# Turning 18 token tiles through DRAM and VectorE's 32 by 32 transpose instead of TensorE, in a kernel of pooled attention and a channel mix

## The reference, cut to what matters

```python
def _attn_ref(q, k, v):                       # q, k, v: 4 x 8 x 1152 x 64
    q_pool = q.reshape(B, H, S // 2, 2, D).mean(axis=3)
    scores = scale * np.matmul(q_pool, k.transpose(0, 1, 3, 2))
    attn = np.exp(scores - np.max(scores, axis=-1, keepdims=True))
    attn = attn / (np.sum(attn, axis=-1, keepdims=True) + 1e-09)
    return np.matmul(attn, v)

def _moe_ref(x, g_ln, w_ch1, w_ch2):          # x: 4 x 576 x 512, w_ch1: 512 x 2048
    mu = np.mean(x, axis=-1, keepdims=True)
    var = np.mean((x - mu) ** 2, axis=-1, keepdims=True)
    xn = (x - mu) / np.sqrt(var + 1e-06) * g_ln
    return x + np.maximum(xn @ w_ch1, 0.0) @ w_ch2
```

## Time and profile before

| what | us |
|---|---|
| median of 3 runs | 806.26 (805.49 to 806.8) |
| the profiled execution: device time | 805.31 |
| the profiled execution: span of the core | 803.5 |
| TensorE busy in the span | 792.1 (99%) |
| VectorE busy | 640.5 (80%) |
| ScalarE busy | 417.4 (52%) |
| POOL busy | 446.0 (56%) |
| DMA traffic | 75.36 MB, mean 94 GB/s |

### The profile page before, as it was taken

The page is one execution under the profiler, slowest core; times in us unless marked ns, Lnnn a source line. Parts: engine busy times, 40 slices in busy tenths (PEclk is TensorE's granted clock), DMA queues, the critical chain, the costliest instruction groups (busy, mean ns, idle before and its releaser), DMA issues. The chain is left out here.

```text
span 803.5 us, 17054 instructions
## 1 busy us (share of the span) xinstructions
PE 792.1 (99%) x6472; PEld 662.9 (83%) x6472; DVE 640.5 (80%) x991; ACT 417.4 (52%) x941; POOL 446.0 (56%) x341
## 2 busy tenths in 40 slices
PE   8999999999999999999999999999999999999998
PEld 6778777787778777788879999989899989999897
DVE  6987889888889989888597767898867888766654
ACT  4677556576556675667723354543244444333431
POOL 3899989888888888787795221331411342131100
PEclk9999999999999999999999999999999999999999
DMA  8566634466534565311112211214212122422112
GB/s 193 130 146 147 143 97 97 105 148 147 119 89 103 131 148 141 69 67 44 32 53 66 93 53 53 66 53 138 85 66 69 58 72 66 154 70 64 55 40 79
DMA packets 39681, 75.36 MB, mean 94 GB/s; under 512 B 8880, under 2 KB 23472, under 8 KB 36016
## 3 DMA queue, kind: packets, MB, share of 16 engines
q1 hardware_dynamic: 38128, 73.88, 35.0%
q10 hardware_dynamic: 1472, 0.39, 0.3%
HBM read 69.54 MB, written 4.72 MB: 92 GB/s over the span
## 5 line engine op out<-in xcount | busy, mean ns | idle before, releaser
L588 POOL TENSOR_TENSOR acc<-acc,pT 128x576 f32<-128x576 f32 x160 | 240.7, 1505 | 23.2 <-ACT pT L932 0.4
L1299 PE MATMUL banks<-w2f,hT 128*128 128x512 f32 x864 | 214.3, 393 | 0.0
L932 ACT ACTIVATE pT<-banks 128x576 f32<-128x576 f32 x288 | 171.8, 658 | 37.0 <-PE banks L726 31.4
L1299 PEld LDWEIGHTS banks<-w2f,hT 128*128 128x128 f32 x864 | 160.3, 188 | 28.8 <-issue 0.2
L1043 DVE TENSOR_REDUCE pm<-banks 128x2 f32<-128x1024 f32 x128 | 153.4, 1222 | 37.5 <-PE banks L672 36.0
L728 PE MATMUL banks<-qT,kT 64*128 64x288 f32 x1728 | 162.0, 298 | 2.4 <-DVE pm L1043 1.8
L728 PEld LDWEIGHTS banks<-qT,kT 64*128 64x128 f32 x1728 | 133.9, 184 | 17.2 <-DVE pm L1043 7.3
L739 PE MATMUL banks<-pT,vn 128*64 128x288 f32 x1152 | 146.1, 408 | 0.0
L1377 ACT ACTIVATE hT<-mid 128x384 fp32r<-128x384 f32 x88 | 46.4, 527 | 182.0 <-DVE mid L1444 181.0
L398 POOL TENSOR_TENSOR w_sums<-w_stage 128x256 f32<-128x256 f32 x22 | 17.7, 806 | 210.9 <-DMA w_stage<-in_moe_w_ch_dram 210.9
L1444 DVE TENSOR_TENSOR mid<-banks,mid 128x384 f32<-128x384 f32 x154 | 85.5, 555 | 59.2 <-PE banks L1288 55.9
(11 more groups left out here) (122 smaller groups left out, 960.9 us busy)
## 6 DMA issues: line engine op xcount, KB each, us to landing
q_in_rows<-in_q_dram SPq DMA_DIRECT2D x56, 284.0 KB, 6.6
k_in_rows<-in_k_dram SPq DMA_DIRECT2D x56, 284.0 KB, 5.1
w_stage<-in_moe_w_ch_dram SPq DMA_DIRECT2D x24, 512.0 KB, 3.8
w_stage<-in_moe_w_ch_dram SPq DMA_DIRECT2D x48, 256.0 KB, 2.7
vn<-in_v_dram SPq DMA_DIRECT2D x16, 576.0 KB, 4.7
out_dram<-x SPq DMA_DIRECT2D x16, 256.0 KB, 3.1
q_in_rows<-in_q_dram SPq DMA_DIRECT2D x4, 256.0 KB, 3.0
k_in_rows<-in_k_dram SPq DMA_DIRECT2D x2, 288.0 KB, 4.0
```

Source lines behind the costliest of these rows:

```text
L588: nc.gpsimd.tensor_tensor(total, pT[:, h % 2, 0] if kt == 1 else total, pT[:, h % 2, kt], ALU.add).then_inc(chained, 1)
L932: nc.scalar.activation(pT[:, h % 2, kt], pair_banks("S", n)[:, :, 0:HW], ACT.Exp, scale=SCALE).then_inc(exp_done, 1)
L1299: last = nc.tensor.matmul(banks[:, k % 2 * (CT // 2) + kk], hT[:, k, a, tokens], w2f[:, (2 * u + k // 2) % 4, b], start=p == 0 and k < 2 a ...
```

## The change

1. TensorE's transpositions of tokens are gone, in attention and in the mix, with the waits around bank 7.
2. In their place, for each tile: SP sends the normalised tile to a DRAM tensor `tokens` (`send_tokens`, 128 rows of 2 KB); when it has landed, SP fetches it with four DMAs of 64 KB (`fetch_blocks`), each to 32 partitions, in pieces of 32 float32 numbers (128 bytes), so that the 32 by 32 blocks stand in transposed places; when these have landed, VectorE turns each block in itself with one STREAM_TRANSPOSE of 128 x 512 (`turn_tokens`), into `xg_a` or `xg_b`. ScalarE multiplies there in place by g (`scale_tokens`). The blocks use the memory of `token_sums`, in three sets.
3. The order of normalising, of the statistics (now two tiles at a time in the units 2 to 4 for the third part, its moments at the end of unit 9), of the power on POOL (one unit earlier) and of the work of the last two pairs of attention on VectorE and ScalarE moves accordingly. The high parts of the forms B12 and B22 of the first part go from VectorE to ScalarE.
4. At the start: 8 of the 28 idle transpositions go, one group of maxima goes ahead of the keys of the second pair, and the second piece of the first keys is loaded by SP behind the first instead of by ScalarE's queue.

```diff
-                  "S@6 M@4 S@0 O@6 E@3 L@0 T@4 PV@2 T@0 KQ@4 KA@6 SH@3 Z@1 PV@0")
+                  "S@6 M@4 S@0 O@6 E@3 L@0 PV@2 KQ@4 KA@6 SH@3 Z@1 PV@0")
-    FIRST_STEPS = "KQ@2 W@7 W@7 KA@0 W@7 M@4 M@6 M@4 W@2 M@6 W@2 M@4 KA@0 M@6 M@2 KQ@4 L@6 W@1 W@1 SF@0"
+    FIRST_STEPS = "KQ@2 W@7 KA@0 M@4 M@6 M@4 W@2 M@6 W@2 M@4 M@6 KA@0 M@2 KQ@4 L@6 W@1 W@1 SF@0"
...
-        def turn_tokens(n, kk, bank):
-            nc.tensor.wait_ge(xn_ready, CT * n + kk + 1)
-            for c in range(DC):
-                last = nc.tensor.transpose(bank[:, c * 128:(c + 1) * 128],
-                                           xn[:, kk % 2, c * 128:(c + 1) * 128], ident[:])
-            last.then_inc(xn_turned, 1)
+        def blocks(t):
+            at = t % BLOCK_SETS * DM
+            return token_sums[:].rearrange("p s c w -> p (s c w)")[:, at:at + DM]
+
+        def send_tokens(sp, n, kk):
+            t = CT * n + kk
+            sp.wait_ge(xn_ready, t + 1)
+            sp.dma_start(tokens[t], xn[:, kk % 2]).then_inc(xn_sent[t % 2], 16)
+
+        def fetch_blocks(sp, n, kk):
+            t = CT * n + kk
+            sp.wait_ge(xn_sent[t % 2], 16 * (t // 2 + 1))
+            wait(sp, tokens_turned, t - BLOCK_SETS + 1)
...
+            for r in range(128 // BLOCK):
+                sp.dma_start(blocks(t)[r * BLOCK:(r + 1) * BLOCK].rearrange("j (c a i) -> j c a i", c=DC, i=BLOCK),
+                             tokens_v[t, r]).then_inc(blocks_in[t % BLOCK_SETS], 16)
+
+        def turn_tokens(n, kk):
+            t = CT * n + kk
+            nc.vector.wait_ge(blocks_in[t % BLOCK_SETS], 64 * (t // BLOCK_SETS + 1))
...
+            nc.vector.transpose(half[:, :, at].rearrange("p c (a j) -> p c a j", j=BLOCK),
+                                blocks(t).rearrange("p (c a i) -> p c a i", c=DC, i=BLOCK)).then_inc(tokens_turned, 1)
...
             first_keys(sp, 0, k_first)
+            first_keys(sp, 1, k_in)
...
-            first_keys(act, 1, k_in)
...
             for u in range(UNITS):
+                n, p = u // FP + 1, u % FP
+                if n < PARTS:
+                    if p == 2:
+                        send_tokens(sp, n, 0)
+                        send_tokens(sp, n, 1)
+                        fetch_blocks(sp, n, 0)
+                        fetch_blocks(sp, n, 1)
+                    elif p in (3, 4):
+                        fetch_blocks(sp, n, 2 * p - 4)
+                        send_tokens(sp, n, 2 * p - 3)
+                        fetch_blocks(sp, n, 2 * p - 3)
                 if u + 2 < UNITS:
                     load_first_weights(sp, u + 2)
...
                 if p == 1 and n > 1:
+                    moments_of(n)
+                    variance_eps(n)
+                if p in (2, 3, 4):
+                    turn_tokens(n, 2 * p - 4)
+                if p in (2, 3):
+                    normalize(n, 2 * p - 2)
+                if 2 <= p < 5 and n + 1 < PARTS:
                     dve.wait_ge(x_written, PAIRS)
-                    for kk in range(4):
-                        statistics(n, kk)
...
-                if p == 2 and n > 1:
-                    statistics(n, 4)
-                    statistics(n, 5)
-                    moments_of(n)
-                    variance_eps(n)
-                if p in (4, 5):
-                    normalize(n, 2 * p - 5)
+                if p == 2:
+                    normalize(n, 0)
+                    normalize(n, 1)
+                if p in (3, 4, 5):
+                    turn_tokens(n, 2 * p - 5)
+                if p in (3, 4):
+                    normalize(n, 2 * p - 3)
```

135 lines of the change are left out of this document (74 added, 61 removed).

## The result

The changed kernel takes 797.38 us, the median of 4 runs (796.51, 797.13, 797.62, 800.43), against 806.0 for the kernel before, the median of its 4 runs. The ratio is 0.9896, 95% interval 0.9881 to 0.9911: 1.0% faster. The forecast was 796.0, its range 794.4 to 799.2. The profiled execution took 796.51 us with a span of 794.8 (before 805.31 and 803.5), so it gained 8.8 us where the sum had 10.3.

What follows compares the result with a forecast made beforehand. TensorE's instruction stream was taken as the bound; gains of 5.3 + 3.8 + 0.8 + 0.4 = 10.3 us, added work hidden, bring 805.3 to 795.0 profiled, 796.0 in the median; 8-in-10 range 794.4 to 799.2.

Steps and rivals of the forecast that it cites:

- forecast case: Whole kernel: the summed gains arrive and the added work stays hidden; 794.5 to 797 us, chance 0.66.
- first rival: Units 2 to 5 and 10: VectorE becomes the bound, costing 3.0 us, so 799.0 us; chance 0.18.
- Transpositions in the mix: Mix: removing 12 tile transpositions at 0.44 us each from TensorE's path gains 5.3 us.
- the statistics: Unit 10: moving the third part's statistics to units with room removes the excess over 15.65 us, gaining 0.8 us.
- Transpositions in attention: Attention: three pairs that turn two tiles each lose 1.27 us at their ends, gaining 3.8 us.
- The start: Program start: four fewer idle transpositions let the first keys be turned sooner, and every later step follows; 0.4 us gained.
- SP's queue: Unit 2: unit 4's first weights, behind sends and fetches, land by 460.8 us plus queueing; 2.3 us to spare, cost nothing.
- Attention keeps its time: Attention's last pairs: late fetches delay maxima twice by 1.3 us, or ScalarE's casts hold the end; 798.6 us, chance 0.06.
- VectorE at nothing: VectorE: 18 added transpositions, 0.65 us each by length, fit its idle time; units 3 and 4 reach 13.5 and 14.9 us busy.
- The way through DRAM: Mix: a tile's send and fetches take 7.3 to 9.5 us, hidden with 0.5 us to spare at the slow end.
- Room on the DMA engines: DMA engines: a tile's 2048 pieces at 22.7 ns take at most 2.9 us, so there is room enough.
- third rival: SP's queue, units 2 to 4 and 10 to 12: small pieces clog the DMA engines, up to 819 us; chance 0.06.

Runs made afterwards that it cites:

- Putting the price back: Changed kernel with four idle TensorE transpositions at each of the 12 places of the mix where a tile was turned before; 806.29 us.
- six-fetch run: Changed kernel with six small fetches instead of four for each of the mix's 12 tiles, VectorE waiting for them too; 807.62 us.
- two kernels with the old list: Changed kernel with the earlier first steps, 797.17 us; the same with last values loaded sooner and one GpSimd add fewer in attention's last half, 797.26 us.
- run with the 2.6 us wait: Changed kernel with the keys of the second pair turned ahead of the sixth group of maxima again; 800.56 us.

## Why the prediction was right, and where it was off

The mechanism of the main sum is shown: what left TensorE's stream left the time. The measured median, 797.38, lies just above the band of the forecast case (794.5 to 797) and in that of the first rival (797 to 799.5), but not by that rival's mechanism: the 1.5 us between sum and profile are the start and the last pair. Of the signs of being right, the units 3 to 5 and 10 to 13 (15.6 to 15.7 us), the ends of the pairs 12 and 13 (10.8 us) and TensorE's waits (8.3 us in total) came as stated.

*Transpositions in the mix, 5.3, and the statistics, 0.8:* right; 6.21 us measured for 6.1. Putting the price back gave 6.4 for the 5.3 (1.0 of it unexplained), and the statistics alone gave their 0.8 in the kernel before.

*Transpositions in attention, 3.8:* right; 3.77. No run put these back; the stretch of the pairs 11 to 14 alone shows it. Comparing the ends of two pairs, instead of counting 2 x 0.44, was what made it so.

*The start, 0.4 gained:* wrong, 0.37 lost in the profiled execution, 0.1 to 0.5 over all profiles at full clock. The step that failed is "Every later step of the start waits for this one". The first maximum did come 0.38 us sooner. But the keys of the second pair already bound the start of the kernel before: they were turned at 13.89, 0.13 us behind their landing. In the change their load is issued 0.23 us sooner, but lands only 0.10 sooner. And the change puts a group of maxima ahead of them, which the prediction gave no price at all; they are turned at 14.47. With the order put back they are turned 0.13 us behind their landing again, never before 13.98, and the first scores follow 5.8 us behind that. That they land 0.1 to 0.3 us later in those runs than at 13.76 isn't explained. A stretch with two inputs gains only what both gain.

*The last pair, costed at nothing:* 0.76 lost. What failed is an omission: SP's queue was followed past the weights of the mix, and not past `load_values(PAIRS - 1)`, which went from 0.44 us behind the end of pair 14 to 8.13 behind it. By itself that made TensorE wait 0.9 us. Taking it away didn't bring the time back, since the turns and the waits for blocks also delay VectorE's low parts and, beside these, GpSimd's sum (26.9 for 26.4). Of the rival "Attention keeps its time" this is what came: nothing in pairs 12 to 14, 0.8 us at the end, and in the changed kernel not by ScalarE's casts.

*VectorE at nothing:* right. 0.70 us a turn, and 8.4 us more of them cost 0.45. Its busy time was counted 1.2 us too high in each unit (12.27 for 13.5 in unit 3, 13.66 for 14.9 in unit 4). The second part of the first rival, that GpSimd's adds stretch two-operand work of VectorE, occurs (4.15 us for two low parts that take 0.95 each elsewhere), and the kernel before had it in the mix too: in unit 4 a `hidden_lo` took 1.09 us and a low part of a weight 0.97 beside GpSimd's sums. With the change's order no `hidden_lo` of that unit takes more than 0.60 us and no low part of a sum more than 0.43, which is most of the 1.2 us. That was luck: the prediction did not see it.

*The way through DRAM:* right for the mix. A send and a fetch land after 2.6 us each (3 to 5 was the sign for the small pieces), and VectorE never waits for blocks there. In the last pair, which the prediction did not follow, it waits 3.0 and 1.9 us for them.

*Room on the DMA engines:* right, with the bound on the high side. In the stretch from 448.2 to 454.5 us, nearly all of it two tiles' fetches (packets, MB, share of 16 engines),

```profile
q1 hardware_dynamic: 3713, 0.57, 50.9%
```

are 0.509 x 6.3 x 16 / 3713 = 13.8 ns a packet, where 22.7 was the bound: 1.8 us of the 16 engines for a tile and not 2.9. (This takes in 59 packets of 2048 bytes; by themselves the packets of 128 bytes average 12.9 ns over the whole run.) The Trainium skill's 512 bytes ("DMA: Bandwidth & Descriptors", Specifications) doesn't decide here: pieces of 128 bytes are indeed slow for their size, 128 bytes in 13.8 ns being 9.3 GB/s for an engine where the 2048-byte packets of this stretch take 86.5 ns, or 23.7 GB/s, but a tile is 2048 of them and no more. A read-modify-write no row here shows.

*SP's queue:* right, and closely. The first weights were to land at 460.8 in the time of the kernel before, with 2.3 us to spare. They landed at 458.34; this place stands 2.6 us earlier now (454.73 for 457.30), so 460.9 by the old time. The six-fetch run puts the room at 2.1. The third rival's sign, ScalarE's casts waiting for their weights in the units 3 and 11, did come (2.9 us in each), and cost nothing: as a sign it was too sharp, since ScalarE has that time to spare. The six-fetch run also shows how near that rival was: 1.3 us more of SP a tile turned a gain of 8.8 us into a loss of 1.8 (one execution, with one stretch at the lower clock in it).

## What to carry to other kernels

When a step is taken off the engine that bounds the kernel, its price can be read from two equal stretches with and without it, and in a steady loop it comes back whole. Where the program changes phase, several inputs arrive just in time, so a sooner one gains nothing until the others are followed too: go through every queue that the new instructions join, list what stands behind them, and find for each step the input that lands last. Many small DMAs may cost the issuing queue more than the DMA engines; the thing to compare is the seconds of issue, here 0.65 us for 64 KB, with the slack of the load behind them.

## What the runs showed of the hardware

*The clock at the start.* The changed kernel ran once with the first scores at 20.08 us and once at 21.94, with the same instructions. In the second run, by stretches (PEclk is the column ahead of the DMA share):

```profile
9.00:12.00 3.00, 2.04 (x12) 1.02 (x12) 2.62 (x3) 2.39 (x7) 0.92 (x1) 1.00 0.80 204
12.00:16.00 4.00, 4.00 (x16) 2.51 (x15) 3.86 (x4) 0.00 (x0) 4.00 (x3) 0.52 0.93 211
16.00:19.00 3.00, 3.00 (x19) 2.55 (x17) 1.65 (x2) 1.93 (x2) 0.57 (x1) 0.51 0.96 197
```

TensorE had idled 0.9 us for VectorE's maxima in the first of these, then the clock fell to the 1.2 GHz level at 12.14 us and rose at 18.97. The run with idle transpositions in the mix shows the same at 11.73 to 18.56. Both have the shortened list of first steps; so do other profiles at full clock, with the same idle 0.9 us, so that idle time alone doesn't decide it. Whether the removed idle transpositions make this likelier is open: eight runs of the two kernels with the old list (796.2 to 798.2) and eight of the changed kernel (796.3 to 800.4) are too few.

*Short waits can cost more than themselves.* TensorE's waits for the last values of 0.9, 1.7, 1.8 and 2.15 us were followed by no lower clock. The waits of 2.6 us there and of 2.4 us in the mix were each followed by 3.4 us at the 1.2 GHz level. The changed kernel's run of 800.43 us has no profile; its mean granted clock, 0.998, is that of the run with the 2.6 us wait (800.56 us), so it may be the same case, which is not shown.

*GpSimd and VectorE slow each other.* One GpSimd add of 128x576 takes 1.4 us, and a low part of VectorE's with two SBUF operands 0.95. Side by side either gets longer: at 390.45 us, after, an add took 2.29 us while the low part beside it kept its 0.94, and from 407.78 on two low parts took 2.05 and 2.16 us and the adds beside them 1.94 and 1.96. The Trainium skill says so ("GPSIMD Engine Reference", Key points: interfaces shared, contention with VectorE instructions in a 2-port perf mode or with two SBUF inputs), and for two inputs these rows agree. VectorE's transpositions keep their 0.70 us beside GpSimd's adds (383.73 us, after). A normalisation, which reads one SBUF tile, takes 0.50 to 0.58 us in the mix and 1.01 beside these adds (382.79), so it isn't the number of inputs alone; whether it runs in the mode that the page names no row shows.
